# A three-stage kernel (attention, MLP, top-1 experts) on one core: beta loaded as one row and spread by TensorE, z loaded by rows and turned by TensorE, the last store placed behind the branch for further experts

## The reference

```python
# attention with a memory: B, H, S, D = 2, 8, 576, 64
scores = q @ k.T / sqrt(D), causal; a = softmax(scores); local = a @ v
q_p = phi(q)                                  # phi(x) = elu(x) + 1
mem_out = (q_p @ M_prev) / (q_p @ z_prev + 1e-6)
g = 1 / (1 + exp(-beta))                      # one beta for each head
x = g * mem_out + (1 - g) * local             # then 1152 tokens of width 512
# MLP: w_in 512 x 2048, w_out 2048 x 512
h = x @ w_in; g = h if h >= 1, 0 if h <= -1, else (h + 1)**2 / 4; x = g @ w_out
# 8 experts, top-1, capacity 288: tokens beyond it give zero
out[i] = gate[i] * (relu(x[i] @ w1[e]) @ w2[e])
```

## Time and profile before

| | |
|---|---|
| time, three runs | 331.07, 331.31, 332.03 us (median 331.31) |
| the profiled execution | 329.83 us, of which its span is 327.9 us |
| instructions | 7012 |
| mean granted clock of TensorE over the span | 0.995 |
| DMA | 77362 packets, 38.46 MB; 68342 packets under 512 B |

### The profile page before, as it was taken

The page is one execution under the profiler, slowest core; times in us unless marked ns, Lnnn a source line. Parts: engine busy times, 40 slices in busy tenths (PEclk is TensorE's granted clock), DMA queues, the critical chain, the costliest instruction groups (busy, mean ns, idle before and its releaser), DMA issues.

```text
span 327.9 us, 7012 instructions
## 1 busy us (share of the span) xinstructions
PE 308.8 (94%) x2714; PEld 249.6 (76%) x2714; DVE 206.8 (63%) x539; ACT 143.7 (44%) x318; POOL 142.2 (43%) x168
## 2 busy tenths in 40 slices
PE   2897999999999999999999999999999999999892
PEld 2465676766766988886999989898989867775771
DVE  4478999899979356897784657647845443531300
ACT  1368578577676344545551442534344322101020
POOL 4047789889989400463780011613160042520111
PEclk9999999999999999999999999999999999999998
DMA  6899669564517710000000309630042085019970
GB/s 116 126 225 220 148 130 230 128 133 150 155 42 173 225 42 2 0 2 2 0 2 9 65 6 387 167 65 1 2 72 38 0 311 205 2 21 391 404 288 7
DMA packets 77362, 38.46 MB, mean 117 GB/s; under 512 B 68342, under 2 KB 68342, under 8 KB 76304
## 3 DMA queue, kind: packets, MB, share of 16 engines
q1 hardware_dynamic: 73904, 36.77, 40.3%
q10 hardware_dynamic: 2400, 0.59, 1.0%
q0 software_dynamic: 1024, 0.64, 0.7%
HBM read 32.67 MB, written 5.43 MB: 116 GB/s over the span
## 4 chain that ended last, share of the span: by engine, by line
PE 85%; DVE 7%; issue 2%; DMA 2%; POOL 2%; ACTq 0%; ACT 0%; POOLq 0%
PE bank_a L1636 14%; PE bank_b L1636 14%; PE bank_out L1593 6%; PE bank_a L1508 4%; PE bank_pt L1695 4%; PE bank_pt L1547 4%; PE bank_b L1695 4%; PE bank_a L1570 3%; PE bank_b L1843 2%; PE bank_b L1852 2%; PE bank_a L1843 2%; PE bank_a L1852 2%; DVE g_raw L1185 2%; PE bank_out L1669 2%; DMA k_rows<-in_k_dram 2%
## 5 line engine op out<-in xcount | busy, mean ns | idle before, releaser
L659 POOL TENSOR_SCALAR prob<-prob,rl,gate_loc 128x512 f32<-128x512 f32 (+3 forms) x64 | 41.5, 662 | 15.0 <-DVE rl L1106 15.0
L1636 PE MATMUL bank_a<-x_hi,win_hi 128*128 128x288 f32 x128 | 39.3, 307 | 0.0
L1636 PE MATMUL bank_b<-x_hi,win_hi 128*128 128x288 f32 x128 | 38.1, 298 | 0.0
L1636 PE MATMUL bank_a<-x_lo,win_hi 128*128 128x288 f32 x128 | 37.8, 296 | 0.0
L1636 PE MATMUL bank_b<-x_lo,win_hi 128*128 128x288 f32 x128 | 37.8, 295 | 0.0
L1636 PE MATMUL bank_a<-x_hi,win_lo 128*128 128x288 f32 x128 | 37.7, 295 | 0.0
L1636 PE MATMUL bank_b<-x_hi,win_lo 128*128 128x288 f32 x128 | 37.7, 294 | 0.0
L831 ACT ACTIVATE prob<-prob,negmax 128x512 f32<-128x512 f32 (+3 forms) x64 | 35.0, 549 | 2.2 <-DVE negmax L1056 2.1
L892 ACT ACTIVATE g_raw<-bank_a,biases 128x576 f32<-128x576 f32 x16 | 11.9, 742 | 51.3 <-DVE sq L1179 51.3
L739 POOL DMA_INDIRECT few_d<-row,slot_l x12 | 12.4, 1030 | 49.7 <-issue 24.4
L1185 DVE TENSOR_TENSOR g_raw<-g_raw,sq 128x576 f32<-128x576 f32 x32 | 31.3, 979 | 2.4 <-ACT sq L893 2.4
(11 more groups left out here) (293 smaller groups left out, 757.2 us busy)
## 6 DMA issues: line engine op xcount, KB each, us to landing
w_sb<-in_moe_w_dram SPq DMA_DIRECT2D x6, 2048.0 KB, 13.3
win_raw<-in_moe_w_in_dram SPq DMA_DIRECT2D x4, 1024.0 KB, 5.8
wout<-in_moe_w_out_dram SPq DMA_DIRECT2D x4, 1024.0 KB, 5.8
win_raw<-in_moe_w_in_dram SPq DMA_DIRECT2D x1, 4096.0 KB, 13.9
out_dram<-zero_row SPq DMA_DIRECT2D x8, 288.0 KB
x_d<-x_rows SPq DMA_DIRECT2D x32, 72.0 KB, 2.0
v_sb<-in_v_dram SPq DMA_DIRECT2D x16, 128.0 KB, 2.4
qn<-in_q_dram SPq DMA_DIRECT2D x24, 72.0 KB, 4.7
```

What stands on the lines that cost most here:

```text
L659: pool.tensor_scalar(prob[u][:, h, :], prob[u][:, h, :], rl[:, c:c + 1], gate_loc[:, 2 * j + h:2 * j + h + 1], ALU.mult, ALU.mult).then_in ...
L1636: last = pe.matmul(h_bank(d)[:, t, :], w[:, m, f:f + P], x[c % 2][:, m, :], start=(m == 0 and n == 0), stop=(m == KT - 1 and n == 2))
```

## The change

Three things. First, `beta` is loaded behind the first loads of q instead of ahead of them, into one partition (a row of 16 numbers); PE multiplies a column of 128 ones by that row (`spread_beta`), which gives it on all partitions in PSUM (`beta_bank`), and ACT's exponential reads it there. Second, z is loaded by ACT's queue, between the loads of `k_rows[0]` and `k_rows[1]`, as 8 rows of 128 numbers (512 bytes each); PE turns it (`turn_z`), and DVE copies it into the two columns of `mz` with two small copies (`copy_z`) behind `copy_q(0)`. The four-byte runs of L494 go away, and M has a semaphore of its own. Both new PE operations stand between `turn_q(0)` and `scores(0, 3)`. Third, POOL's indirect store of `y_few` moves behind `jobs_of`, with a semaphore of its own (`s_last`), and `y_few` now lies on the place of `zero_row`, so that DVE waits for the zero stores (`s_clear`) before it writes it.

```diff
-        gate_in, _, _ = sb("gate_in", [P, BH], F32)
+        gate_in, _, _ = sb("gate_in", [1, BH], F32)
+        z_rows, _, _ = sb("z_rows", [NPAIR, 2 * D], F32)
...
+        y_few, _, _ = sb("y_few", [P, DM_PART], F32, at=zero_at)
...
-        STATIC = 16 * (slot_tiles + 1)
+        STATIC = 16 * slot_tiles
...
+        beta_bank, z_bank = bank_pt[1][:, 0:BH], bank_pt[0][:, 0:NPAIR]
...
                     sp.dma_start(mz[part, :, D * h:D * h + D], m3.rearrange("(i h) d e -> h d i e", h=2)[h:h + 1, :, :, :]
-                                 .rearrange("a d i e -> (a d) i e")).then_inc(s_z, 16)
-                    sp.dma_start(mz[part, :, 2 * D + h:2 * D + h + 1], z3.rearrange("(i h) (d o) -> h d i o", h=2, o=1)[h:h + 1, :, :, :]
-                                 .rearrange("a d i o -> (a d) i o"), allow_slow_non_contiguous=True).then_inc(s_z, 16)
+                                 .rearrange("a d i e -> (a d) i e")).then_inc(s_m, 16)
...
-            sp.dma_start(gate_in[:, :].rearrange("p (b h) -> p b h", b=B),
-                         beta.rearrange("(a c h) -> a c h", a=1, c=1).broadcast_to([P, B, H])).then_inc(s_beta, 16)
             load_tiles(sp, q_rows[0], q3[0:2, :, :], s_qrow[0])
+            sp.dma_start(gate_in[0:1, :].rearrange("p (b h) -> p b h", b=B),
+                         beta.rearrange("(a c h) -> a c h", a=1, c=1).broadcast_to([1, B, H])).then_inc(s_beta, 16)
...
             def work(n):
 
+                sp.wait_ge(s_kye, 1)
...
-            pool.wait_ge(s_kye, 1)
-            pool.wait_ge(s_fid, 7)
-            pool.indirect_dma_start(out=pieces[:, :], out_offset=bass.IndirectOffsetOnAxis(ap=few_id[:, 0:1], axis=0),
-                                    in_=y_few[:, :], in_offset=None, bounds_check=GROUPS * N - 1, oob_is_err=False).then_inc(s_out, 16)
-
...
             jobs_of(pool, work)
+            pool.wait_ge(s_kye, 1)
+            pool.wait_ge(s_fid, 7)
+            pool.indirect_dma_start(out=pieces[:, :], out_offset=bass.IndirectOffsetOnAxis(ap=few_id[:, 0:1], axis=0),
+                                    in_=y_few[:, :], in_offset=None, bounds_check=GROUPS * N - 1, oob_is_err=False).then_inc(s_last, 16)
+            pool.wait_ge(s_last, 16)
             pool.wait_ge(s_out, STATIC)
...
-            for n in range(2):
-                load_tiles(act, k_rows[n], k3[2 * n:2 * n + 2, :, :], s_krow[n])
-
-            act.wait_ge(s_beta, 16)
-            act.activation(gate_mem[:, :], gate_in[:, :], ACT.Exp, scale=-1.0).then_inc(s_gates, 1)
+            load_tiles(act, k_rows[0], k3[0:2, :, :], s_krow[0])
+            act.dma_start(z_rows[:, :], z3.rearrange("(i h) d -> i (h d)", h=2)).then_inc(s_z, 16)
+            load_tiles(act, k_rows[1], k3[2:4, :, :], s_krow[1])
+
+            act.wait_ge(s_bt, 1)
+            act.activation(gate_mem[:, :], beta_bank, ACT.Exp, scale=-1.0).then_inc(s_gates, 1)
...
+            def copy_z():
+
+                dve.wait_ge(s_zt, 1)
+                for h in range(2):
+                    part = slice(D * h, D * h + D)
+                    dve.tensor_copy(mz[part, :, 2 * D + h], z_bank[part, :]).then_inc(s_zc, 1)
+
...
             copy_q(0)
+            copy_z()
             row_max(0, 3)
...
+            dve.wait_ge(s_clear, 16 * (NPAIR + 2))
             dve.wait_ge(s_ky, 1)
             dve.tensor_copy(y_few[:, :], bank_o[:, 0:DM_PART]).then_inc(s_kye, 1)
...
+            def spread_beta():
+
+                pe.wait_ge(s_const, 9)
+                pe.wait_ge(s_beta, 16)
+                pe.matmul(beta_bank, ones_f[0:1, :], gate_in[0:1, :], start=True, stop=True).then_inc(s_bt, 1)
+
+            def turn_z():
+
+                pe.wait_ge(s_z, 16)
+                pe.transpose(z_bank, z_rows[:, :], ident[0:NPAIR, 0:NPAIR]).then_inc(s_zt, 1)
+
...
-                    pe.wait_ge(s_z, 64)
+                    pe.wait_ge(s_m, 32)
+                    pe.wait_ge(s_zc, 2)
...
             turn_q(0)
+            spread_beta()
+            turn_z()
```

More of the change, by code:

```diff
@@ L95, in build_program @@
         ones_f, _, _ = sb("ones_f", [1, P], F32)
-        zero_row, _, _ = sb("zero_row", [N // NPAIR // 2, DM], F32)
+        zero_row, zero_at, _ = sb("zero_row", [N // NPAIR // 2, DM], F32)
         SLOTS_P = E * SLOTS // ST
@@ L235, in build_program @@
         h_fewT = [sb(f"h_fewT{k}", [P, 2, P], F32)[0] for k in range(OTHERS + 1)]
-        y_few, _, _ = sb("y_few", [P, DM_PART], F32)
         assert offset[0] <= later_at
@@ L268, in build_program @@
         s_kt = sem("s_kt")
+        s_m = sem("s_m")
         s_z = sem("s_z")
+        s_zt = sem("s_zt")
+        s_zc = sem("s_zc")
+        s_bt = sem("s_bt")
         s_v = [sem(f"s_v{p}") for p in range(2)]
@@ L343, in build_program @@
         s_out = sem("s_out")
+        s_last = sem("s_last")
         s_tabf = sem("s_tabf")
```

## The result

| | before | after |
|---|---|---|
| median (lowest to highest, runs) | 331.19 us (330.58 to 332.03, 4) | 328.17 us (327.92 to 328.41, 4) |
| ratio of after to before | | 0.991, 95% interval 0.988 to 0.993 |
| the profiled execution, its span | 329.83, 327.9 us | 328.41, 326.6 us |

The changed kernel is 3.0 us faster, 0.9%.

A forecast was written before the change was run, and what follows sets the result against it. The prediction took k's landing, held up by beta's load, to bound the start while PE sets the pace afterwards. A gain of 3.0 less 0.3 for the clock, 0 elsewhere, took 331.31 to 328.6 us, range 326.9 to 331.2.

The forecast's parts named there:

- What bounds the start, and why k lands late: Start: k's landing at 8.58 us sets PE's start; beta's pieces, all reading the same 32 bytes, pass slowly ahead of it.
- K's landing: Start: k lands at 5.6 us instead of 8.58, a gain of 3.0, with bounds of 1.6 and 4.4.
- Added work and waits at nothing: Start: the two PE products, DVE copies and waits for z and beta cost nothing, 0.2 as the products' other end.
- The clock: PE's rise from 1.2 to 2.4 GHz near 17.5 us: at an unmoved rise half the gain is lost; 0.3 taken off.
- The end at nothing: End: moving POOL's last store gains nothing, with bounds of 0.5 gained and 0.1 lost.
- Rival 3: End: POOL's drain goes with the jump, up to 2.4 us more gained, 326.2 us; chance 0.04.
- Sum: Whole kernel: 3.0 - 0.3 + 0 = 2.7 us gained, profiled execution 327.1 us, median 328.6 us.
- 1: Start: a program's first reads are slow whoever makes them; only 0.0 to 0.9 us saved, 330.9 us; chance 0.20.
- 2: PE's clock rises later than before; a delay of 3.5 us costs 1.2 us, 332.5 us; chance 0.06.
- 4: Start: k comes sooner, but PE's new wait for z and beta ends near 12.2 us, 331.0 us; chance 0.04.

The follow-up runs named there:

- e7_fill: Kernel before with beta's change alone, plus fifteen instead of ten identity transposes ahead of k's: 326.73 us, ratio 0.988.
- e4_same: Kernel before with beta's change alone, plus an unread load ahead of q, 256 pieces of 32 bytes from the same 32 bytes of beta: 329.51 us, one execution.
- e4_distinct: Kernel before with beta's change alone, plus an unread load ahead of q, 256 pieces of 32 bytes from 256 places of q: 326.79 us, one execution.
- e6_row_first: Kernel before with beta's change alone, but the one-row load ahead of q instead of behind it: 327.52 us, one execution.
- e2: Kernel before with the change of z alone, by rows on ACT's queue, turned by PE, copied by DVE: 330.99 us, ratio 1.001.
- after_again: The whole changed kernel once more, for a second profile, against the kernel before: 328.36 us, ratio 0.993.
- before_again: The kernel before, unchanged, once more for a second profile: 329.55 us, one execution.
- e1_again: Kernel before with beta's change alone (one row behind q, spread by PE), run a second time: 327.16 us, ratio 0.992.
- e3: Kernel before with only the store of `y_few` moved behind `jobs_of`, with `s_last`, and `y_few` on `zero_row`'s place: 331.52 us, ratio 1.0027.
- e5: Kernel before with the old 256-piece beta load placed behind q's loads, nothing else: 327.39 us, ratio 0.991.

## Why the prediction was right

- **What bounds the start, and why k lands late.** Right, and shown: the load of k ends PE's wait ahead of k's transposes in each kernel but e7_fill, where that pause is filled, and beta's pieces hold both queues back at the start because they read the same bytes (e4_same against e4_distinct, with the reserve on the two tensors told there).
- **K's landing.** Predicted 5.6 with 4.2 to 7.0; measured 5.82 in the profile of after and 5.52 to 5.81 in the other executions with the row behind q. Its two terms were off to opposite sides, which is luck in a small way: the packets were taken to be through at 4.6 and were by 4.4 (2337 passed from 1.8 on, 1151 of them of k's queue), and the lag from there to the landing, for which 1.0 was a choice between two bounds, was 1.4. That q competes with k in beta's place, for which the Trainium skill was cited, is seen in the first 1.5 us, with 800 packets of q beside 525 of k, and in e6_row_first, where q comes later, 802 of k pass and k is turned from 5.40.
- **Added work and waits at nothing.** Right: both products end 0.17 before q's copy does, and e2 measures z's part at 1.001.
- **The clock.** Set at a loss of 0.3. The mechanism, half of each shift, was right. The size and even the sign depend on which executions are compared, by the lead at the scores and at `memory(0)`: beside before, a gain of 0.27 in after (3.03 for 2.76) and 0.65 in after_again (3.71 for 3.06); beside before_again, a loss of 0.39 in after (2.45 for 2.84), nothing in after_again (3.13 for 3.14), and a loss of 1.03 in e1_again (2.07 for 3.10). The moment moves by 1 to 2 us between executions of one kernel, so the honest term was a range, from about a loss of 1.0 to a gain of 0.7.
- **The end at nothing.** Right for the store: 0.82 against 0.81, the reading was beside it. Rival 3 falls: the drain is 2.445 us with the jump long taken.
- **Sum.** 3.0 - 0.3 = 2.7 was predicted; 2.76 + 0.27 = 3.03 stands at `memory(0)` of the first pair of profiles, and the medians differ by 3.0. That the agreement is this close is partly luck, since the clock alone moves it by more. The sum was made against the profiled time, though, where it gives 327.1 and the execution took 328.41: the stall near 310 us took 1.45 of it, which no step had. It isn't tied to the earlier start, as e2 and e3 have it too.
- **The rivals.** 1 would have needed q10's first packets near 3.3: they came at 2.19, and at 1.97 behind 256 other small pieces. 2 needed a later rise: it came at 12.8 to 15.2 in the executions with the earlier work and at 15.8 to 18.3 in the others, earlier in all, though only 0.6 lies between the two groups. 4 needed PE to wait for z: it waits 0.23 for q's copy.

What the prediction missed is how little of the change the gain needs: e5 shows that exchanging two statements gives it whole, and that z's part and the store's bring nothing here; alone, the store's even measures 0.3% slower.

## What to carry to other kernels

Look at what lies ahead of the first operands in each queue, by packets and not by bytes: here 8 KB that all partitions fetch from the same 32 bytes put off the landing of the first 288 KB of k by 2.8 to 3.2 us. Place such a load behind the loads that the first work waits for, or load it once and spread it on the chip; one of the two was enough here. And read a gain of 1% at the same instruction in both traces, since a pair of whole profiled times can be 1.5 us off by a stall that comes and goes between executions of one kernel. One profile of each is little even then: two executions of the kernel before stand 0.6 apart at `memory(0)`, by the clock alone.

## What the runs showed of the hardware that I had not expected

- 256 pieces of 32 bytes with one source let 110 to 126 packets pass in 1.5 us; 256 such pieces with different sources, together with q and k, 1403. Both queues are held back in that stretch, and the load of k is 3.2 us longer (6.83 against 3.65).
- Five more transposes in a pause bring the rise of PE's clock from near 14 to before 8.0 and before 5.8 us, and in both profiles the clock then fell to 1.2 GHz again for 3.4 us. The rise itself differs by 1 to 2 us between executions of the same kernel.
- POOL's drain at the end of the program is 2.445 us in every profile, with the jump just ahead of it or 14 us earlier.
